# A linear-attention kernel whose opening part is put in another order: first blocks stored and fetched behind the first transposes, the third k's halves and w_out around the first inverse's way

## The reference, cut to what matters

```python
# q, k, v: (4, 8, 768, 48) float32; beta: (4, 8, 768)
k_n = k / (norm(k) + 1e-06)
state = 0                                    # (B, H, D, D)
for t in range(S):                           # delta rule, 768 steps
    y[t] = q[t] @ state
    state += beta[t] * outer(k_n[t], v[t] - state.T @ k_n[t])
x = y as (3072, 384)
h = x @ w_in; g = maximum(0.01 * h, h)       # w_in 384 x 2048
x = g @ w_out                                # w_out 2048 x 384
# then: skip where x @ w_skip <= 0, else the best of 8 experts by x @ w_gate:
# x + prob * (relu(x @ w1[e]) @ w2[e])       # w1[e] 384 x 1024, w2[e] 1024 x 384
```

## Time and profile before

| | |
|---|---|
| median of 3 runs | 953.1 us (952.8 to 955.27) |
| the profiled execution | 950.53 us, of which 948.8 us are the span of the trace |
| PE busy | 805.5 us (85%) |
| DVE busy | 644.0 us (68%) |
| ACT busy | 502.7 us (53%) |
| POOL busy | 412.1 us (43%) |
| mean granted PE clock | 0.944 of full speed |

### The profile page before, as it was taken

The page is one execution under the profiler, slowest core; times in us unless marked ns, Lnnn a source line. Parts: engine busy times, 40 slices in busy tenths (PEclk is TensorE's granted clock), DMA queues, the critical chain, the costliest instruction groups (busy, mean ns, idle before and its releaser), DMA issues.

```text
span 948.8 us, 27901 instructions
## 1 busy us (share of the span) xinstructions
PE 805.5 (85%) x10858; PEld 650.3 (69%) x10859; DVE 644.0 (68%) x1303; ACT 502.7 (53%) x1099; POOL 412.1 (43%) x500
## 2 busy tenths in 40 slices
PE   0314869899999999998989999999984899999986
PEld 0214648787777778787868777778753687788864
DVE  5478868787877778787877787765566835523372
ACT  4436546667575766566665657454453624322161
POOL 4404334536262635344453624253223655644463
PEclk9856699999999999999999999999995999999998
DMA  8774654575667766647656465332363943611100
GB/s 240 128 217 64 121 106 89 109 112 103 121 120 111 132 108 126 122 88 128 111 114 114 87 110 110 68 66 56 86 249 105 321 174 104 228 66 45 38 24 16
DMA packets 309830, 109.97 MB, mean 116 GB/s; under 512 B 284930, under 2 KB 301364, under 8 KB 309344
## 3 DMA queue, kind: packets, MB, share of 16 engines
q1 hardware_dynamic: 304000, 94.63, 48.0%
q0 software_dynamic: 3232, 7.64, 2.3%
q10 hardware_dynamic: 2496, 6.29, 1.8%
HBM read 60.39 MB, written 20.46 MB: 85 GB/s over the span
## 4 chain that ended last, share of the span: by engine, by line
PE 37%; DVE 24%; ACT 14%; issue 13%; DMA 6%; SPq 3%; POOL 2%; DVEq 1%; ACTq 0%; POOLq 0%
PE b_acc L807 8%; PE b_acc L681 8%; PE b_h L791 7%; PE b_h L668 7%; DVE stage L1294 5%; PE b_ch L606 4%; ACT ga L826 3%; ACT stage L937 3%; DVE inv L1230 2%; DVE inv L1224 2%; ACT stage L826 2%; ACT operands L826 2%; DMA natq<-x_dram,id_in 2%; ACT z L826 2%; DVE inv L1213 1%
## 5 line engine op out<-in xcount | busy, mean ns | idle before, releaser
L1604 POOL TENSOR_TENSOR stage<-stage 128x256 f16<-128x256 f32 x192 | 138.3, 720 | 289.5 <-ACT stage L826 288.6
L681 PE MATMUL b_acc<-wt,stage 128*128 128x384 f16 x1152 | 222.7, 331 | 6.2 <-ACT stage L826 5.7
L668 PE MATMUL b_h<-stage,wt 128*128 128x256 f16 x1728 | 221.7, 274 | 4.4 <-DVE stage L1294 3.2
L668 PEld LDWEIGHTS b_h<-stage,wt 128*128 128x128 f16 x1728 | 159.8, 98 | 24.6 <-DVE stage L1294 4.5
L681 PEld LDWEIGHTS b_acc<-wt,stage 128*128 128x128 f16 x1152 | 107.5, 98 | 63.2 <-POOL stage L1604 8.8
L826 ACT ACTIVATE stage<-stage 128x256 f16<-128x256 f32 x192 | 80.0, 417 | 125.5 <-DVE stage L1294 125.5
L1294 DVE SCALAR_TENSOR_TENSOR stage<-b_h,stage 128x256 f32<-128x256 f32 x192 | 80.9, 421 | 72.4 <-ACT stage L937 72.1
L807 PE MATMUL b_acc<-wt,operands 128*128 128x384 f16 x576 | 101.6, 327 | 6.0 <-DVE operands L1522 6.0
L791 PEld LDWEIGHTS b_h<-y,wt 128*128 128x128 f16 x1728 | 100.6, 100 | 8.3 <-issue 6.4
L791 PE MATMUL b_h<-y,wt 128*128 128x128 f16 x1728 | 103.3, 223 | 3.2 <-DVE y L1157 2.8
L572 PE MATMUL b_gr<-operands 128*128 128x128 f16 x576 | 45.1, 235 | 52.3 <-DMA operands<-operands 21.1
(11 more groups left out here) (174 smaller groups left out, 1300.9 us busy)
## 6 DMA issues: line engine op xcount, KB each, us to landing
operands<-in_moe_w_dram SPq DMA_DIRECT2D x16, 1536.0 KB, 7.0
a_sys<-a_dram SPq DMA_DIRECT2D x24, 256.0 KB, 4.2
natq<-in_q_dram SPq DMA_DIRECT2D x24, 192.0 KB, 4.0
raw_v<-in_v_dram SPq DMA_DIRECT2D x24, 192.0 KB, 3.7
stage<-y SPq DMA_DIRECT2D x96, 48.0 KB, 2.1
x_dram<-stage SPq DMA_DIRECT2D x24, 192.0 KB, 2.9
out_dram<-stage SPq DMA_DIRECT2D x24, 192.0 KB, 3.0
natk<-in_k_dram SPq DMA_DIRECT2D x22, 192.0 KB, 3.9
```

The source lines that it names most:

```text
L668: mm = pe.matmul(b_h[f % 2][:, 0:GT], wt[0][:, a, d * FF + f * P:d * FF + (f + 1) * P], xT[:, g % 2, b, d, :], start=(i == 0), stop=(i == ...
L681: mm = pe.matmul(b_acc[w][:, 0:DM], g16[:, f % 4, a, w * P:(w + 1) * P], wt[1][:, b, f * DM:(f + 1) * DM], start=(f == 0 and (a, b) == PAR ...
L1604: pool.tensor_tensor(g16[:, f % 4, LO, :], g32[:, f % 4, :], g16[:, f % 4, HI, :], ALU.subtract).then_inc(g_lo, 1)
```

## The change

It reorders the prologue and the first turn, and leaves all other turns as they are (`k_part` for later groups is untouched).

- SP: `blocks_out(0)` and `blocks_back(0)` stand right behind `turn_k(0)`; `turn_k(1)` ahead of `turn_q(0)`; `load_k(2)` and `load_q(1)` behind these; `inverse_out(0)`, `inverse_back(0)` ahead of `blocks_out(1)`, `blocks_back(1)`.
- The second half of the first `kn`'s LO part is written by DVE instead of POOL.
- ACT: `kn_high(0)` ahead of `squares(1)`; `gram_out(0)` ahead of `kn_high(1)` and `seed(0)`; all three `split_w_in` and `load_w_out` ahead of `gram_out(1)`; `squares(2)` ahead of `inverse_high(0)`, and `root(2)`, `kn_high(2)`, `seed(1)`, `q_high(1)` behind it.
- DVE: `norm_sum(2)` and `norm(2)` behind the first inverse.
- POOL: `kn_low(2)` in the prologue between the `p_low(0)`, no longer in turn 0; the memsets of `tT` and `a21` ahead of `nat_k(1)`.
- Turn 0: the norms and halves of group 3 in slots 9 to 14 instead of 6 to 11; no links of the second inverse in slots 0 to 2, more in 4 to 7; `q_low(1)` in slots 6 and 7 instead of 4 and 5. `gram_p` has a further wait, because `squares` writes in its buffers.

```diff
-        SECOND = (2, 2, 2, 2, 3, 3, 2, 0, 0, 0, 6, 6, 5, 0, 0, 0)
+        SECOND = (0, 0, 0, 2, 4, 5, 4, 1, 0, 0, 6, 6, 5, 0, 0, 0)
...
             return dict(squares=3, sum=5, root=6, norm=7, scale=8, split=8)[what] if g else dict(
-                squares=6, sum=7, root=7, norm=8, scale=9, split=9)[what]
+                squares=9, sum=10, root=10, norm=11, scale=12, split=12)[what]
...
@@ SP
             turn_k(0)
+            blocks_out(0)
+            blocks_back(0)
+            turn_k(1)
             turn_q(0)
-            turn_k(1)
             load_k(2)
             load_q(1)
-            blocks_out(0)
-            blocks_back(0)
             load_v(0)
...
+            inverse_out(0)
+            inverse_back(0)
             blocks_out(1)
             blocks_back(1)
-            inverse_out(0)
-            inverse_back(0)
...
@@ ACT, turn
-                    if g == 0 and f in (0, 1):
-                        kn_high(2, f)
@@ ACT, prologue
+            for x in range(2):
+                kn_high(0, x)
             squares(1)
             root(1)
-            for x in range(2):
-                kn_high(0, x)
+            split_w_in(0)
             for x in range(2):
                 q_high(0, x)
+            for st in range(B):
+                gram_out(0, st)
+            for x in range(2):
+                kn_high(1, x)
             act.wait_ge(const_pool, 1)
             seed(0)
-            split_w_in(0)
-            for x in range(2):
-                kn_high(1, x)
-            for st in range(B):
-                gram_out(0, st)
             a21_high(0)
             split_w_in(1)
-            squares(2)
-            root(2)
+            split_w_in(2)
+            load_w_out()
             for st in range(B):
                 gram_out(1, st)
-            load_w_out()
-            split_w_in(2)
+            squares(2)
+            inverse_high(0)
+            root(2)
+            p_high(0, 0)
+            p_high(0, 1)
+            split_w_out(0)
+            for x in range(2):
+                kn_high(2, x)
+            for st in range(2, B):
+                p_high(0, st)
+            act.wait_ge(wg_loaded, 32)
+            copy(wg16[:, HI], wg[:], GW_S).then_inc(wg_hi, 1)
+            split_w_out(1)
+            for i in range(2, 4):
+                split_w_out(i)
+            seed(1)
             for x in range(2):
                 q_high(1, x)
-            act.wait_ge(wg_loaded, 32)
-            copy(wg16[:, HI], wg[:], GW_S).then_inc(wg_hi, 1)
-            inverse_high(0)
-            p_high(0, 0)
-            split_w_out(0)
-            seed(1)
-            p_high(0, 1)
-            split_w_out(1)
-            for st in range(2, B):
-                p_high(0, st)
-            for i in range(2, 4):
-                split_w_out(i)
...
@@ DVE
+                if st == 0:
+                    dve.wait_ge(n2_ready, min(g + 3, G))
...
-                    if g == 0 and f in (4, 5):
-                        q_low(1, f - 4)
+                    if g == 0 and f in (6, 7):
+                        q_low(1, f - 6)
...
+            dve.wait_ge(kn_hi, 2)
+            dve.tensor_tensor(kn[0][C:P, LO, :, C:C + D], natk[C:P], kn[0][C:P, HI, :, C:C + D], ALU.subtract
+                              ).then_inc(kn_ready, 1)
...
-            norm_sum(2)
-            norm(2)
             split_w_in(1)
             inverse(0, 0, LINKS)
             inverse_low(0)
-            split_w_in(2)
+            norm_sum(2)
+            norm(2)
             dve.wait_ge(const_pool, 1)
             dve.wait_ge(beta_ready, 1)
             gram_p(0, 0)
             gram_p(0, 1)
+            split_w_in(2)
             split_w_out(0)
             gram_p(0, 2)
             gram_p(0, 3)
-            split_w_out(1)
             dve.wait_ge(wg_hi, 1)
             lo(wg16[:, LO], wg[:], GW_S, wg16[:, HI]).then_inc(wg_ready, 1)
+            split_w_out(1)
...
@@ POOL
-                    if g == 0 and f in (1, 2):
-                        kn_low(2, f - 1, up_at(g, f - 1))
...
-            for g in range(2):
-                nat_k(g)
-                for x in range(2):
-                    kn_low(g, x, None)
+            nat_k(0)
+            kn_low(0, 0, None)
+            pool.wait_ge(kn_ready, 2)
             pool.memset(tT.bitcast(F32), 0.0)
             link(pool.memset(a21.bitcast(F32), 0.0))
             pool.sem_inc(const_pool, 1)
+            nat_k(1)
+            for x in range(2):
+                kn_low(1, x, None)
             pool.dma_start(spare_dram, row_id[:]).then_inc(yo_scattered, 16)
+            for st in range(2):
+                p_low(0, st)
             nat_k(2)
-            for st in range(B):
+            for x in range(2):
+                kn_low(2, x, None)
+            for st in range(2, B):
                 p_low(0, st)
```

More of the change, by code:

```diff
@@ L1446, in _ @@
             zeros(nq16)
+            dve.wait_ge(kn_hi, 2)
+            dve.tensor_tensor(kn[0][C:P, LO, :, C:C + D], natk[C:P], kn[0][C:P, HI, :, C:C + D], ALU.subtract
+                              ).then_inc(kn_ready, 1)
+            zeros(kn[1])
             norm_sum(1)
-            zeros(kn[1])
             norm(1)
+            split_w_in(0)
             for x in range(2):
                 q_low(0, x)
-            split_w_in(0)
             zeros(kn[2])
```

## The result

The changed kernel takes 963.7 us (961.8 to 966.6, 4 runs) where the kernel before took 954.2 in the runs beside it: ratio 1.0109, 95% interval 1.0086 to 1.0132. (The ratios in this text are estimates over all runs; the quotient of two medians, here 1.0100, differs from them by up to 0.001, about 1 us.) The forecast was 952.8 with a range of 948.0 to 958.6, so the time lies outside it, on the slow side. Of the two profiled executions, 966.6 us is the highest of the changed kernel's four runs and 950.5 lies under all four of the kernel before, so their distance of 16.1 us is more than that of the medians; I use them for places, and the ratios for sizes.

What follows compares the result with a forecast made beforehand. From 137 us PE is busy; before that DVE and its partners set the pace, so the start of `scan_u` of group 1 counts. -5.9 + 0.2 + 4.9 + 0.5 = -0.3 us: 952.8 against 953.1, range 948.0 to 958.6.

Steps and rivals of the forecast that it cites:

- the load of w_out against SP's queue: Prologue: w_out flows 9.1 us, to 49.1, ahead of half of `turn_q(0)` and `load_k(2)`, which lands at 54.
- the 57: Prologue: sign of a slower result, ACT starting `inverse_high(0)` after 57 us; forecast 54.9.
- the load of k decides: Prologue rival: slow DMA makes `load_k(2)` land late, up to 6 us; 958.1 us, chance 0.18.
- The list behind the first inverse: Prologue: work behind the first inverse takes from 54.9 to the first `scan_u` at 77.2, using 7.6 us of 13.5 won.
- The scan of group 0: Turn 0, first `scan_u` to `inverse_low(1)`: DVE's work about the same, net +0.2 us, between -1.5 and +3.
- SP's detour: Turn 0: `load_k(4)` waits for `kn` 3 ahead of `inverse_out(1)`, delaying `scan_u(1)`; +4.9 us, from 3.1 to 6.5.
- The clock: Before `scan_u(1)`: PE idle some 7 us, not 4.10, costs at most 1.6 us of pulses; taken as 0.5.
- First transposes at nothing: Prologue: `turn_k(0)` issued at about 13.7, not 16.99, but first `gram_a` stays at 23.1; no gain.
- The bundled rule: Prologue rival: engines drain bundles per queue, `load_k(2)` lands about 6 us sooner; 951.8 us, chance 0.05.
- -5.9: End of the prologue: the first `scan_u` starts at 77.2 against 83.14, 5.9 us earlier.

Runs made afterwards that it cites:

- a5: The changed kernel with POOL's small store moved to slot 2 of turn 1; 961.5 us, 1.0073 of the kernel before.
- b2: The kernel before with POOL's small store moved to slot 2 of turn 1; 948.2 us, 0.9930 of before.
- a4: The changed kernel with `load_k(2)` ahead of `turn_k(1)` on SP; 964.8 us, 1.0100 of the kernel before.
- d1: c2 with w_out's load early again, as in the change; 954.6 us, 0.9994 of the kernel before.
- c2: The changed kernel with w_out's load behind `gram_out(1)`, group 3's norm in its old slots and the small store in turn 1; 948.1 us, 0.9932 of before.
- a2: The changed kernel with group 3's norm and halves back in their old slots of turn 0; 960.0 us, 1.0052 of the kernel before.
- b1: The kernel before with group 3's norm and halves in the late slots and the added `gram_p` wait; 960.7 us, 1.0068 of before.
- c3: c2 with `q_low(1)` back in slots 4 and 5 of turn 0; 947.5 us, 0.9919 of the kernel before.
- c4: c3 with the links of the second inverse spread as before, from slot 0 on; 948.6 us, 0.9928 of the kernel before.
- e1: The kernel before with the small store's 512 bytes taken from one partition, same place and queue; 948.9 us, 0.9920 of before.
- e2: The kernel before with POOL's small store in turn 1 and a four-byte-piece copy issued by SP behind `turn_k(1)`; 958.1 us, 1.0028 of before.
- a1: The changed kernel with POOL's small store right behind the constants; 966.6 us, 1.0121 of the kernel before.

## Why the prediction was wrong

**The step that failed** is "the load of w_out against SP's queue". It had `load_k(2)` landed at 54; ACT could start `squares(2)` only at 63.4, and `inverse_high(0)` at 64.18, far behind the 57 that the prediction gave as its own sign of being wrong. Two things are in the 9.4 us. The crawl behind the small store is one, which the sum had at nothing and only a rival priced (a5 takes it away: 60.0; by the ratios 3.4 us; in the old order, where it lies in the first blocks' store, it is worth 6.7, b2). The other 6 are a mis-sized term. In a5 w_out's data ends at 52.5, not 49.1: it starts 0.6 later and takes 11.8 us, not 9.1, a length that I had taken from its fastest microsecond. Behind it the transposes need until 56.0, not 1.9 us as forecast but 3.5, because `turn_k(1)` was still in the queue: I had it through before w_out, and did not count its 4,096 pieces from the moment when `a_sys` was. The last microsecond lies between the load's last piece and `squares(2)`, 2 us where I had 1. Hence `gram_a(1)` and with it `gram_out(1)`, both ahead of `inverse_high(0)` on ACT, were late too, which no step of mine had: in the changed kernel they alone would have held ACT until 59.2, so the load of k was not the only limit, and a4, which put it first, gained nothing. d1 against c2 puts the early load of w_out at 5.9 us with nothing else in play, and c2, with neither, starts its first `scan_u` at 75.34, even before the 77.2 of the forecast.

**The rival "the load of k decides"** named the place, the crawl and the condition, with 958.1 and a chance of 0.18. It was right in kind and too small. Its argument against itself, that transposes inside the core may not suffer from the crawl, fell: `turn_k(1)` crawled just like loads (282 packets in 5 us). Its 958.1 left out that w_out would be slow as well. I had two rows that said the store and the crawl go together and should have given them more weight.

**The list behind the first inverse** was forecast as 22.3 us from `inverse_high(0)` to the first `scan_u`; it took 23.5 (64.18 to 87.69). Right, with 1.2 missing: `nat_k(2)` took 2.98 us where I had 1.47, and `kn_high(2)` waited for it.

**The scan of group 0** was to bring +0.2 and brought +3.5: from the first `scan_u` to the end of `inverse_low(1)` 47.0 us instead of 43.5. Of this 2.7 belong to the late slots, which I had let cost nothing there (a2 against the changed kernel; 1.4 of it is `inverse_low(1)` beside POOL's `kn_low(3)`, and b1 shows 2.4 without the rest). The links out of slots 0 to 2 cost 3.3 where I had 1 to 2 (c3 against c4), and c4, which has them back and `kn_low(2)` in the prologue, needs 41.6 us against the 43.5 of before, so the latter gives about the 1 to 2 of the forecast. `turn_q(1)` landed only at 117.96 and PE waited 4.59 us for it where I had allowed up to 1; but c3 takes a wait of 2.43 of this kind away from c2 and gains nothing that can be told, so it seems not to be on the way that decides. These sizes come from single traces.

**SP's detour** was the best step, with some luck in the sum. Forecast 4.9; from the end of `inverse_low(1)` to `scan_u` of group 1 it was 14.4 instead of 10.5 us, and with the 1.4 above this makes 5.4, which a2 also gave; b1 gave 6.5 in the other kernel. `inverse_out(1)` came 2.6 us behind `inverse_low(1)`, not 4, because that one had itself become longer, which I had not foreseen; the store behind k and `a_sys` took 1.9 us more.

**The clock** was put at 0.5. The turn behind 149.16, which answers to the one behind 137 in the earlier trace rows:

```profile
149.16:202.00 52.84, 50.20 (x702) 40.41 (x702) 38.44 (x86) 32.23 (x79) 22.92 (x25) 0.94 0.56 107
```

0.94 against 0.97, which is up to 1.6 us. From this `scan_u` to that of group 2 it is 53.1 us against 51.9 in the kernel before, 1.2 more. That can't be put down to the longer wait: over the sixteen traces this stretch takes 51.9 to 54.0 us, 53.3 in b2, whose slots are the old ones. The 4.0 us by which all that follows `scan_u` of group 1 is longer also lie within what the traces show there, 811.4 to 816.1.

**First transposes at nothing**: right (the "second from 19 on" of that step is a microsecond). `turn_k(0)` was issued at 14.44, 2.6 earlier, took 6.63 us to issue, and `gram_a` started 0.14 sooner.

**The bundled rule** of the Trainium skill (DMA: Bandwidth & Descriptors, "Queues, rings and completion order") doesn't describe these two queues: 208 pieces of w_out against 212 of a transpose in one microsecond, as before the change. Such equal counts alone would also fit equal bundles on both sides. But in the ten steps of 0.1 us from 60 to 61 of the kernel before, each has 20 to 25 pieces of w_out and 20 to 25 small ones; nine pieces of w_out in a row would keep an engine for six such steps (65 ns each), and 16 engines that did so would swing far more. The same section of the Trainium skill has each engine take turns between its queues, and that the trace shows.

By terms, in the two traces: -5.9 became +4.6, +0.2 became +3.5, +4.9 became +4.0 (its other 1.4 is in the term ahead), and 0.5 became 1.2, if that is its place at all. The first three make the 12.0 us at `scan_u` of group 1; by all runs the change costs 10.4 (8.2 to 12.6), 9.5 by the medians. The first is the miss.

## What to carry to other kernels

When work is moved into a gap, ask what had filled that gap for others: here the wait for the first inverse had covered a norm, a load and two transposes, and the gain of 14 us at the first link became a wait of 12 behind the last. In these kernels a load that is issued early on one queue is paid by everything small on the other queue, piece by piece; count pieces, from the moment when the queue is free for them, not from their issue, and time a transfer over its whole flow, not over one microsecond of it. A store of a few bytes per partition deserves a look at any place of a prologue: moved, or written as one run, it was worth 6.7 us or more, the reordering of the whole front 3.6 at its best, and nothing once the store was out of the way.

The best of these kernels are b2, c2, c3, c4 and e1, 0.992 to 0.993 of before; that e1's one line can be joined with c3 was not tried.

## What the runs showed of the hardware that was not expected

A store of 512 bytes to DRAM, four bytes from each of 128 partitions, brings the DMA engines nearly to a halt for some 4 to 8 us. The halt begins about 2 us after the issue in e2, 3.5 in the kernel before, 5 in the changed one and 7 in a1. It comes whether POOL (before: 809 packets in 6 us) or SP (e2: 588) issues the store, and holds transposes between two places in the core as well as loads. The same number of bytes out of one partition does not do this (e1: 4,026, with nothing left to do from 41 on). That the store has 128 pieces is read from the program; the trace shows 32 packets on POOL's queue in either form.

Two queues with work share the engines one piece for one piece at all sizes seen here: 8,192 bytes against 192 (before, 11 to 12: 58 packets against 58), and 1,536 against 128 or 256. So 2,048 pieces of 1,536 bytes held the small pieces of the other queue to about 210 a microsecond for most of 11.8 us, where they move at over 1,000 alone (1,129 in the earlier trace rows).

A VectorE instruction can be held by one of GpSimd: `inverse_low(1)`, two of 128x256, takes 1.22 us, and 2.66 with POOL's `kn_low(3)` of 1.64 us beside it.
